# Windowed attention into a mixture of experts: v loaded once and shifted on chip, x's sums and rests on one engine

## The chip, the cores and the metric

One core of one Trainium2 chip runs the whole kernel in one launch. The metric is the device time in microseconds (us) of that launch. The engines are TensorE (PE), VectorE (DVE), ScalarE (ACT), GpSimd (POOL) and the queue of SyncE (SP), which issues every transfer.

## The reference, cut to what matters

q, k and v have the shape (4, 8, 576, 64); the mixture has 2304 tokens, model width 512, 8 experts and a hidden width of 1024. Everything is float32.

```python
scores = scale * np.matmul(q, k.transpose(0, 1, 3, 2))
rel = pos[:, None] - pos[None, :]
scores = np.where((rel >= 0) & (rel < 64), scores, -1e9)
attn = softmax(scores)                       # max subtracted, + 1e-9 in the sum
x = (attn @ v).transpose(0, 2, 1, 3).reshape(2304, 512)

logits = x @ w_gate;  P = np.exp(logits - logits.max())
for _ in range(8):                           # rows, then columns
    P /= P.sum(1, keepdims=True) + 1e-9
    P /= P.sum(0, keepdims=True) + 1e-9
    P *= N / E
for e in range(8):
    out += P[:, e:e+1] * (np.maximum(x @ w1[e], 0.0) @ w2[e])
```

## The kernel before, in words

**Attention.** The work goes in 16 pairs p of heads, four pairs to a batch entry. A pair has 9 blocks of 64 queries; a block sees its own 64 keys and the 64 before them. TensorE makes the scores of a pair, ACT copies the own half out of PSUM (`own`), VectorE merges in the half before and takes the row maximum (`merge`), POOL subtracts it (`shift`, L716), ACT takes the exponential (`exp`), VectorE the sum and its reciprocal (`soften`), POOL multiplies and writes each probability twice, side by side (`weigh`, L724). TensorE transposes the result (L321), VectorE masks the transposes into `p_t` (`turned`, L796), and TensorE multiplies by `v_win` (`mix`, L331). ACT copies the product into `x_raw` (`x_copy`, L553).

`v_win` holds for each block 128 rows of v: the own 64 keys on partitions 64 to 127 and the 64 before on partitions 0 to 63. So one pair's v is loaded twice, by L240 (288 KB) and, shifted by a block, by L241 (256 KB). It has two buffers; the load of pair p waits for the mix of pair p - 2.

**Order.** Each engine has its own list, written by hand, and works through it strictly in order. TensorE's turn p (`attend`) is the scores of p, the mix of p - 3 and the transposes of p - 2. POOL's turn p is `shift(p)`, `weigh(p - 1)`, and a piece of extra work. ACT's turn p is `exp(p - 1)`, `own(p)`, `x_copy(p - 3)`, and extra work. VectorE's is `turned(p - 3)`, `merge(p)`, `soften(p - 1)`, and extra work. SP issues q and k of pair p + 3, then v of pair p - 1, and in turns 4, 8 and 9 the weights of the first two tiles.

**The extra work.** The products x @ w1 are Strassen products in Winograd's form: seven (P1, P6, P2, P7, P5, P4, P3 in the order in which TensorE wants them) of quarter matrices. For x they need the sums T1 to T4 (`x_sum`, L705) beside P1, P2 and P3, which are parts of x itself. Each of the seven operands is split into a high part (`x_split`, a cast on ACT, L537) and a rest (`x_rest`, operand minus high part); likewise each tile of weights, with four sums (`sums`, L672 to L677), one split (`w1_split`, L520) and rests (`w1_rest`, L682). x comes in three superblocks s of 768 tokens: superblock 0 needs pairs 0 to 7 in full, and P1 and P2 of it only the first 384 tokens, which pairs 0 to 3 give. Here the rests of superblock 0 are made on VectorE (L817) in turns 12, 14, 15 and after, the sums T1 to T4 on POOL in turns 11 to 14, the sums of the first two weight tiles on POOL in turns 5 and 8.

**The seam.** After turn 16 TensorE does P1 and P6 of the first tile, turn 17 (mix of 14, transposes of 15), P2 and P7, the mix of 15, P5 and P4, the gate product over all of x, P3, and the transposes of the logits. From there 96 weight tiles (3 superblocks, 8 experts, 4 tiles each) run at TensorE's pace. On ACT the seam is: `exp(15)`, `x_copy(13)`, `p1_copy(0)`, the split of the second weight tile, `x_copy(14)`, `relu_11`, `x_copy(15)`, the other relus.

Of the kernel before, what the change touches and what calls it, by code (L numbers as in the profile page):

```python
# [12 lines left out]
P = 128  # L13
# [37 lines left out]
A11, A12, A22, S1, S2, S3, S4 = range(7)  # L51
OF_W = {P1: A11, P6: S2, P2: A12, P7: S3, P5: S1, P4: A22, P3: S4}
T1, T2, T3, T4 = range(4)
XRING = 10
BLK = 2 * P
RAW = 8 * BLK
# [2 lines left out]
def build(nc, qk, v, w_gate, w1, w2, consts, out):  # L59
    with ExitStack() as ctx:  # L60
# [78 lines left out]
        pads_set = sem("pads_set")  # L139
        qk_loaded = [sem(f"qk_loaded{i}") for i in range(QKR)]  # L140
        v_loaded = [sem(f"v_loaded{i}") for i in range(2)]
        scores_done = sem("scores_done")
        own_taken = sem("own_taken")
        scores_taken = sem("scores_taken")
# [84 lines left out]
        def _(sp):  # L229
# [6 lines left out]
            def load_v(p):  # L236

                if p >= 2:
                    sp.wait_ge(x_done, p - 1)
                sp.dma_start(v_win[WINDOW:P, p % 2, :, :], v[p]).then_inc(v_loaded[p % 2], 16)  # L240
                sp.dma_start(v_win[0:WINDOW, p % 2, 1:QB, :], v[p, :, 0:QB - 1, :]).then_inc(v_loaded[p % 2], 16)  # L241

            def load_w1(f, slot, done):

# [55 lines left out]
        def _(pe):  # L300
# [22 lines left out]
                last.then_inc(transposed, 1)  # L323

            def mix(p):
                pe.wait_ge(v_loaded[p % 2], (p // 2 + 1) * 32)
                pe.wait_ge(p_t_ready, p + 1)
                for i in range(QB):
                    for h in range(2):
                        c = slice(h * D, (h + 1) * D)  # L330
                        last = nc.tensor.matmul(ps_x[c, i * WINDOW:(i + 1) * WINDOW], v_win[:, p % 2, i, c],  # L331
                                                p_t[:, i, c], start=True, stop=True)
                last.then_inc(x_done, 1)
# [38 lines left out]
            def product(s, n, slot, k):  # L372

                x, y = bank[slot], bank[1 - slot]
                if k == P1:
                    pe.wait_ge(w1_lo_ready, n + 1)
                    wait(pe, h_ready, n * 4 - 1)
                    o, opens = x, True
                elif k == P6:
                    wait(pe, h_ready, n * 4)  # L380
                    o, opens = y, True
                elif k == P2:
                    pe.wait_ge(p1_out, n + 1)
                    o, opens = x, False
                elif k == P7:
                    pe.wait_ge(u2_done, n + 1)
                    o, opens = y, True
                elif k == P5:
                    pe.wait_ge(h_ready, n * 4 + 1)
                    o, opens = x, True  # L390
                elif k == P4:
                    pe.wait_ge(u3_done, n + 1)
                    o, opens = y, False
                else:
                    pe.wait_ge(h_ready, n * 4 + 2)
                    o, opens = x, True
                if s is not None:
                    pe.wait_ge(xv_lo_ready, s * PRODUCTS + k + 1)
                return o, opens

            def multiply(s, first, n, slot, k):
# [114 lines left out]
        def _(act):  # L516
# [11 lines left out]
            def x_split(s, k):  # L528
                if k in (P1, P2, P3):
                    if s == 0:  # L530
                        act.wait_ge(x_taken, 2 * PAIRS)
                else:
                    act.wait_ge(t_done, s * 4 + {P5: 1, P6: 2, P7: 3, P4: 4}[k])
                if s and k >= XRING - PRODUCTS:

                    act.wait_ge(prod_done, PRODUCTS * (s * PER_SB - 1) + (k - (XRING - PRODUCTS)) + 1)
                nc.scalar.copy(xv_hi[:, x_slot(s, k), :, :], x_operand(s, k)).then_inc(xv_hi_ready, 1)  # L537
# [6 lines left out]
            def own(p):  # L544
                act.wait_ge(scores_done, p + 1)
                wait(act, probs_ready, p - SCR + 1)
                nc.scalar.copy(sc[:, p % SCR, :, :], ps_s[:, :, WINDOW:KEYS]).then_inc(own_taken, 1)

            def x_copy(p):
                act.wait_ge(x_done, p + 1)  # L550
# [62 lines left out]
            for p in range(NP):  # L613
                if p:
                    exp(p - 1)
                own(p)
                if p >= 3:
                    x_copy(p - 3)
                if p == 6:
                    w1_split(0, 0, 0)  # L620
                if p == 11:
                    x_split(0, P1)
                if p == 13:
                    x_split(0, P6)
                    x_split(0, P2)
                if p == 14:
                    x_split(0, P7)
                    x_split(0, P5)
                if p == 15:
                    x_split(0, P4)  # L630
                    x_split(0, P3)
            exp(NP - 1)
            x_copy(NP - 3)
            p1_copy(0, 0)
            w1_split(1, 1, 0)
            x_copy(NP - 2)
# [25 lines left out]
        def _(pool):  # L662
# [30 lines left out]
            def x_sum(s, i):  # L693

                if s:
                    pool.wait_ge(xv_lo_ready, s * PRODUCTS)
                else:
                    pool.wait_ge(x_taken, 2 * PAIRS)
                b11, b12 = (x_raw[:, s, 0:2, h * HT:(h + 1) * HT] for h in range(2))
                b21, b22 = (x_raw[:, s, 2:4, h * HT:(h + 1) * HT] for h in range(2))  # L700
                if i in (T2, T4):
# [2 lines left out]
                        T4: (b21, t_raw[:, T2, :, :])}[i]  # L704
                nc.gpsimd.tensor_tensor(t_raw[:, i, :, :], a, b, ALU.subtract).then_inc(t_done, 1)  # L705

            def x_rest(s, k):
                pool.wait_ge(xv_hi_ready, s * PRODUCTS + k + 1)
                at = x_slot(s, k)
                nc.gpsimd.tensor_tensor(xv_lo[:, at, :, :], x_operand(s, k), xv_hi[:, at, :, :].bitcast(F32),  # L710
                                        ALU.subtract).then_inc(xv_lo_ready, 1)
# [19 lines left out]
            for p in range(NP):  # L731
                shift(p)
                if p:
                    weigh(p - 1)
                if p == 5:
                    sums(0, 0, 16)
                if 6 <= p < 11:
                    w1_rest(0, 0, p - 6, p - 5)
                if p == 8:
                    sums(1, 1, 16)  # L740
                if p == 10:
                    w1_rest(0, 0, 5, 7)
                if 11 <= p < 15:
                    x_sum(0, p - 11)
            weigh(NP - 1)
            w1_rest(1, 1)
            w2_rest(0, 0)
            sums(2, 0, landed(2))
# [43 lines left out]
        def _(dve):  # L792
# [14 lines left out]
            def soften(p):  # L807
# [2 lines left out]
                nc.vector.tensor_reduce(soft_sum[:, k, :], sc[:, k, :, :], AX_X, ALU.add).then_inc(sum_done, 1)  # L810
                dve.wait_ge(sum_done, p + 1)
                nc.vector.reciprocal(soft_inv[:, k, :], soft_sum[:, k, :]).then_inc(inv_done, 1)

            def x_rest(k):
                dve.wait_ge(xv_hi_ready, k + 1)
                at = x_slot(0, k)
                nc.vector.tensor_tensor(xv_lo[:, at, :, :], x_operand(0, k), xv_hi[:, at, :, :].bitcast(F32),  # L817
                                        ALU.subtract).then_inc(xv_lo_ready, 1)

            def rest(n, slot, o, f, half, i):  # L820
                dve.wait_ge(h_hi_ready, n * 4 + i + 1)
# [151 lines left out]
            for p in range(NP):  # L973
# [2 lines left out]
                merge(p)  # L976
                if p:
                    soften(p - 1)
                if p == 12:
                    x_rest(P1)  # L980
                if p == 14:
                    x_rest(P6)
                    x_rest(P2)
                if p == 15:
                    x_rest(P7)
                    x_rest(P5)
            turned(NP - 3)
            soften(NP - 1)
            x_rest(P4)
            x_rest(P3)  # L990
            add_u2(0, 0)
            turned(NP - 2)
            rest(0, 0, bank[0], 0, 0, 0)
# [76 lines left out]
```

## Time and profile before

| | us |
|---|---|
| median of 3 runs (lowest, highest) | 1644.83 (1643.73, 1647.8) |
| the profiled execution | 1645.22 |
| its span | 1643.3 |
| PE busy | 1600.0 |
| POOL busy | 995.5 |
| DVE busy | 744.2 |
| ACT busy | 526.7 |

Transfers of the attention stage, by line: q and k 576 KB a pair, median 9.5 us from issue to landing; v 288 KB a pair, 5.7 us, and 256 KB a pair, 8.1 us; weights 512 KB each.

Times of the trace count from the start of the span. The engines' busy times overlap, so they don't add up to the span. A row that ends in a bracket tells how long the engine sat idle before it, and what ended the idle time; "issue" there means that nothing in the profile shows what it waited for. The chain of waits follows the last instruction back to what released it. "PEclk" is the clock that the throttle granted to TensorE, as a part of full speed.

### The profile page before, as it was taken

Reading aid. Unit: us, or ns where it says so; the run is one execution under the profiler, and the core shown is the slowest. Engines: PE = TensorE matmul, PEld = TensorE weight load, DVE = VectorE, ACT = ScalarE, POOL = GpSimd, SP = SyncE. Lnnn points to the kernel's source line nnn. Section 1 sums busy time; section 2 is a strip of 40 time slices with the busy share of each in tenths; the row PEclk is TensorE's granted clock in tenths of the full one; section 3 lists DMA queues with packets and bytes.
Section 4 is the critical chain, followed back from the end, with each engine's and each line's share of the span. In section 5 each row is a group of like instructions: output and inputs, shape, how many; then the busy total and the mean of one; then the engine's idle time right before and its main releaser. Section 6 shows DMA issues by size and latency. Waiting matters only on the chain.

```text
span 1643.3 us, 24260 instructions
## 1 busy us (share of the span) xinstructions
PE 1600.0 (97%) x8880; PEld 1431.1 (87%) x8880; DVE 744.2 (45%) x1263; ACT 526.7 (32%) x753; POOL 995.5 (61%) x644
## 2 busy tenths in 40 slices
PE   7778999999999999999999999999999999999999
PEld 6667888888888888988888889888888898898888
DVE  5667734434344344344344344344344344344343
ACT  2432233233332333333323333334232333332321
POOL 4855455656656778566565565687655656656552
PEclk9989999999999999999999999999999999999999
DMA  8922112112122122121221211213212122121111
GB/s 232 223 67 77 51 53 78 60 68 77 51 77 71 56 77 98 70 77 51 77 75 53 77 56 72 77 51 102 88 54 77 54 74 77 51 77 71 57 64 38
DMA packets 35436, 124.58 MB, mean 76 GB/s; under 512 B 4160, under 2 KB 4416, under 8 KB 35392
## 3 DMA queue, kind: packets, MB, share of 16 engines
q1 hardware_dynamic: 35392, 123.99, 23.1%
q8 instruction: 28, 0.46, 0.1%
q14 instruction: 16, 0.13, 0.0%
HBM read 119.26 MB, written 4.72 MB: 75 GB/s over the span
## 4 chain that ended last, share of the span: by engine, by line
PE 93%; DVE 3%; POOL 2%; issue 1%; DMA 1%; ACT 0%; SPq 0%; POOLq 0%; DVEq 0%
PE ps L428 16%; PE ps L429 16%; PE ps L427 16%; PE ps L411 14%; PE ps L407 14%; PE ps L409 14%; PE ps L309 1%; DMA qk_buf<-qk 1%; POOL probs L724 1%; PE ps L321 1%; PE ps L331 1%; DVE xv_lo L817 0%; DVE row_sum L939 0%; POOL sc L716 0%; DVE p_t L796 0%
## 5 line engine op out<-in xcount | busy, mean ns | idle before, releaser
L682 POOL TENSOR_TENSOR w_lo<-w_raw,w_hi 128x1792 fp32r<-128x1792 f32 (+1 forms) x101 | 391.5, 3877 | 532.3 <-ACT w_hi L520 531.4
L562 ACT ACTIVATE h_hi<-ps 128x384 fp32r<-128x384 f32 x384 | 189.3, 493 | 961.5 <-DVE ps L841 450.4
L428 PE MATMUL ps<-w_lo,h_hi 128*128 128x512 f32 x1152 | 456.9, 397 | 0.0
L429 PE MATMUL ps<-w_hi,h_lo 128*128 128x512 f32 x1152 | 456.5, 396 | 0.0
L427 PE MATMUL ps<-w_hi,h_hi 128*128 128x512 f32 x1152 | 455.0, 395 | 1.3 <-POOL w_lo L689 1.3
L407 PE MATMUL ps<-xv_hi,w_hi 128*128 128x384 f32 x1344 | 450.8, 335 | 1.9 <-DVE h_lo L823 1.0
L411 PE MATMUL ps<-xv_hi,w_lo 128*128 128x384 f32 x1344 | 452.2, 336 | 0.0
L409 PE MATMUL ps<-xv_lo,w_hi 128*128 128x384 f32 x1344 | 449.9, 335 | 0.0
L823 DVE SCALAR_TENSOR_TENSOR h_lo<-ps,h_hi 128x384 fp32r<-128x384 f32 x384 | 214.2, 558 | 366.6 <-ACT h_hi L562 365.8
L407 PEld LDWEIGHTS ps<-xv_hi,w_hi 128*128 128x128 f32 x1344 | 253.4, 189 | 32.0 <-DVE h_lo L823 1.4
L409 PEld LDWEIGHTS ps<-xv_lo,w_hi 128*128 128x128 f32 x1344 | 253.2, 188 | 29.1
L429 PEld LDWEIGHTS ps<-w_hi,h_lo 128*128 128x128 f32 x1152 | 216.7, 188 | 50.3
L689 POOL TENSOR_TENSOR w_lo<-w_raw,w_hi 128x1024 fp32r<-128x1024 f32 x96 | 230.3, 2399 | 49.7 <-ACT w_hi L525 48.6
L411 PEld LDWEIGHTS ps<-xv_hi,w_lo 128*128 128x128 f32 x1344 | 253.0, 188 | 0.0
L427 PEld LDWEIGHTS ps<-w_hi,h_hi 128*128 128x128 f32 x1152 | 216.9, 188 | 24.6 <-POOL w_lo L689 1.6
L428 PEld LDWEIGHTS ps<-w_lo,h_hi 128*128 128x128 f32 x1152 | 216.9, 188 | 23.0
L520 ACT CAST w_hi<-w_raw 128x1792 fp32r<-128x1792 f32 x96 | 162.9, 1697 | 10.8 <-POOL w_raw L677 10.8
L829 DVE TENSOR_TENSOR u<-ps,p 128x384 f32<-128x384 f32 x96 | 53.5, 558 | 214.3 <-PE ps L411 205.1
L838 DVE TENSOR_TENSOR u<-ps,u 128x384 f32<-128x384 f32 x96 | 53.5, 558 | 139.2 <-PE ps L411 138.8
L525 ACT CAST w_hi<-w_raw 128x1024 fp32r<-128x1024 f32 x96 | 99.9, 1041 | 0.0
L834 DVE TENSOR_TENSOR u<-ps,u 128x384 f32<-128x384 f32 x96 | 53.5, 557 | 102.2 <-PE ps L411 102.2
L861 DVE SCALAR_TENSOR_TENSOR x_raw<-ps,prob,x_raw 128x512 f32<-128x512 f32 x126 | 92.1, 744 | 9.8 <-PE ps L429 9.8
(74 smaller groups left out, 949.9 us busy)
## 6 DMA issues: line engine op xcount, KB each, us to landing
w_raw<-w SPq DMA_DIRECT2D x192, 512.0 KB, 3.9
qk_buf<-qk SPq DMA_DIRECT2D x16, 576.0 KB, 9.5
v_win<-v SPq DMA_DIRECT2D x16, 288.0 KB, 5.7
out<-x_raw SPq DMA_DIRECT2D x18, 256.0 KB, 2.3
v_win<-v SPq DMA_DIRECT2D x16, 256.0 KB, 8.1
const_sb<-consts SPq DMA_DIRECT2D x1, 176.0 KB, 3.5
wg<-w_gate SPq DMA_DIRECT2D x1, 64.0 KB, 5.5
```

The costliest lines, as they stand in the source:

```text
L407: nc.tensor.matmul(o, w1_hi[:, slot, c], xv_hi[:, at, kk, :], start=(opens and kk == 0), stop=False, skip_group_check=not opens)
L409: nc.tensor.matmul(o, w1_hi[:, slot, c], xv_lo[:, at, kk, :], start=False, stop=False, skip_group_check=not opens)
L411: last = nc.tensor.matmul(o, w1_lo[:, slot, c], xv_hi[:, at, kk, :], start=False, stop=(kk == 1), skip_group_check=not opens)
L427: nc.tensor.matmul(ps_y[t], h_hi[slot][:, f, c], w2_hi[slot][:, f, :], start=opens, stop=False)
L428: nc.tensor.matmul(ps_y[t], h_hi[slot][:, f, c], w2_lo[slot][:, f, :], start=False, stop=False)
L429: last = nc.tensor.matmul(ps_y[t], h_lo[slot][:, f, c], w2_hi[slot][:, f, :], start=False, stop=closes)
L520: nc.scalar.copy(w1_hi[:, slot, :], w1_raw[:, slot, BLK:RAW]).then_inc(w1_hi_ready, 1)
L525: nc.scalar.copy(w2_hi[slot][:].rearrange("p f d -> p (f d)"), w2_raw[:, slot, :])\
L562: nc.scalar.activation(h_hi[slot][:, f, half * HT:(half + 1) * HT], o, ACT.Relu)\
L682: last = nc.gpsimd.tensor_tensor(w1_lo[:, slot, c], w1_raw[:, slot, (lo + 1) * BLK:(hi + 1) * BLK], w1_hi[:, slot, c].bitcast(F32), ALU.su ...
L689: nc.gpsimd.tensor_tensor(w2_lo[slot][:].rearrange("p f d -> p (f d)"), w2_raw[:, slot, :], w2_hi[slot][:].rearrange("p f d -> p (f d)").b ...
L823: nc.vector.scalar_tensor_tensor(h_lo[slot][:, f, c], o, 0.0, h_hi[slot][:, f, c].bitcast(F32), ALU.max, ALU.subtract).then_inc(h_ready, 1)
```

## The change

- SP no longer issues L241. ACT gets `v_shift(p)`: it copies blocks 0 to 7 of `v_win` from partitions 64 to 127 to blocks 1 to 8 on partitions 0 to 63, once v of pair p has landed and the mix of p - 2 is done. It stands behind `x_copy(p - 1)` in turn p + 2; the mix of p waits for it.
- The rests of superblock 0 leave VectorE and go to POOL. P1 and P2 are split in turns 7 and 8, from the first four pairs, and their rests made in turns 8 and 9. T1 to T4 are in turns 10, 11, 13 and 15, the rests of P5 and P6 in turns 12 and 14, those of P7, P3 and P4 after the last `weigh`.
- The sums of the first weight tile go from turn 5 to 3, its rest from turns 6 to 10 to turns 4 to 6 in two, two and three blocks. The sums of the second tile go from turn 8 to behind the last rest of x.
- The probabilities are written twice, as before.

```diff
@@ the order in which the rests of superblock 0 come ready
+X_TURN = [P1, P2, P5, P6, P7, P3, P4]
@@ SP
                 sp.dma_start(v_win[WINDOW:P, p % 2, :, :], v[p]).then_inc(v_loaded[p % 2], 16)
-                sp.dma_start(v_win[0:WINDOW, p % 2, 1:QB, :], v[p, :, 0:QB - 1, :]).then_inc(v_loaded[p % 2], 16)
@@ TensorE, mix and product
-                pe.wait_ge(v_loaded[p % 2], (p // 2 + 1) * 32)
+                pe.wait_ge(v_loaded[p % 2], (p // 2 + 1) * 16)
+                pe.wait_ge(v_shifted, p + 1)
...
-                    pe.wait_ge(xv_lo_ready, s * PRODUCTS + k + 1)
+                    pe.wait_ge(xv_lo_ready, s * PRODUCTS + (k if s else X_TURN.index(k)) + 1)
@@ ACT
-                        act.wait_ge(x_taken, 2 * PAIRS)
+                        act.wait_ge(x_taken, 2 * PAIRS if k == P3 else PAIRS)
...
+            def v_shift(p):
+                act.wait_ge(v_loaded[p % 2], (p // 2 + 1) * 16)
+                wait(act, x_done, p - 1)
+                nc.scalar.copy(v_win[0:WINDOW, p % 2, 1:QB, :], v_win[WINDOW:P, p % 2, 0:QB - 1, :])\
+                  .then_inc(v_shifted, 1)
...
                 if p >= 3:
                     x_copy(p - 3)
-                if p == 6:
+                if p >= 2:
+                    v_shift(p - 2)
+                if p == 4:
                     w1_split(0, 0, 0)
-                if p == 11:
-                    x_split(0, P1)
-                if p == 13:
-                    x_split(0, P6)
-                    x_split(0, P2)
-                if p == 14:
-                    x_split(0, P7)
-                    x_split(0, P5)
-                if p == 15:
-                    x_split(0, P4)
-                    x_split(0, P3)
+                if p in (7, 8):
+                    x_split(0, (P1, P2)[p - 7])
+                if 11 <= p < 15:
+                    x_split(0, (P5, P6, P3, P7)[p - 11])
             exp(NP - 1)
+            x_split(0, P4)
+            v_shift(NP - 2)
             x_copy(NP - 3)
+            v_shift(NP - 1)
             p1_copy(0, 0)
             w1_split(1, 1, 0)
             x_copy(NP - 2)
@@ POOL
-            def x_rest(s, k):
-                pool.wait_ge(xv_hi_ready, s * PRODUCTS + k + 1)
+            def x_rest(s, k, nth=0):
+                pool.wait_ge(xv_hi_ready, s * PRODUCTS + (nth or k + 1))
...
-                    pool.wait_ge(x_taken, 2 * PAIRS)
+                    pool.wait_ge(x_taken, PAIRS + 2 if i == T1 else 2 * PAIRS)
...
-                if p == 5:
+                if p == 3:
                     sums(0, 0, 16)
-                if 6 <= p < 11:
-                    w1_rest(0, 0, p - 6, p - 5)
+                if 4 <= p < 7:
+                    w1_rest(0, 0, (0, 2, 4)[p - 4], (2, 4, 7)[p - 4])
                 if p == 8:
-                    sums(1, 1, 16)
+                    x_rest(0, P1, 1)
+                if p == 9:
+                    x_rest(0, P2, 2)
                 if p == 10:
-                    w1_rest(0, 0, 5, 7)
-                if 11 <= p < 15:
-                    x_sum(0, p - 11)
+                    x_sum(0, T1)
+                if p == 11:
+                    x_sum(0, T2)
+                if p == 12:
+                    x_rest(0, P5, 3)
+                if p == 13:
+                    x_sum(0, T3)
+                if p == 14:
+                    x_rest(0, P6, 4)
+                if p == 15:
+                    x_sum(0, T4)
             weigh(NP - 1)
+            x_rest(0, P7, 6)
+            x_rest(0, P3, 6)
+            x_rest(0, P4, 7)
+            sums(1, 1, 16)
             w1_rest(1, 1)
             w2_rest(0, 0)
@@ VectorE: x_rest and its calls in turns 12, 14, 15 and after the last soften are gone
```

## Rows read from the trace of the kernel before

**Rows 1.** The page, busy us, share of the span and instructions of each engine

```profile
PE 1600.0 (97%) x8880; PEld 1431.1 (87%) x8880; DVE 744.2 (45%) x1263; ACT 526.7 (32%) x753; POOL 995.5 (61%) x644
```

**Rows 2.** Stretches: length; PE, PEld, DVE, ACT, POOL busy; PEclk, DMA share, GB/s

```profile
60.00:70.00 10.00, 7.70 (x138) 6.95 (x135) 7.37 (x10) 4.04 (x8) 9.82 (x9) 1.00 1.04 232
...
90.00:100.00 10.00, 4.30 (x45) 3.82 (x45) 9.93 (x9) 2.69 (x4) 6.96 (x4) 0.66 0.22 56
```

**Rows 3.** The chain of waits in the attention stage: start, us, what

```profile
70.32 2.94 issue
...
86.74 4.61 DVE xv_lo L817 x2
...
96.09 2.86 DVE xv_lo L817
```

**Rows 4.** TensorE in order of time: start, us, operation, idle before

```profile
15.99 3.56 PE L309 MATMUL ps<-qk_buf 64*64 64x64 f32 x36 [4.07 <-DMA qk_buf<-qk]
...
21.70 2.08 PE L309 MATMUL ps<-qk_buf 64*64 64x64 f32 x36 [1.02 <-DMA qk_buf<-qk]
...
26.46 2.08 PE L309 MATMUL ps<-qk_buf 64*64 64x64 f32 x36
...
30.80 2.08 PE L309 MATMUL ps<-qk_buf 64*64 64x64 f32 x36
...
114.44 1.27 PE L331 MATMUL ps<-p_t,v_win 128*64 128x64 f32 x36 [1.48 <-DVE p_t L796]
```

**Rows 5.** A stretch of half a microsecond, columns as in rows 2

```profile
103.50:104.00 0.50, 0.50 (x5) 0.50 (x4) 0.50 (x1) 0.00 (x0) 0.42 (x1) 0.50 0.84 203
```

**Rows 6.** POOL in order of time

```profile
26.18 1.15 POOL L716 TENSOR_TENSOR sc<-sc,row_max 128x576 f32<-128x576 f32 x1 [1.02 <-DVE row_max L805]
...
38.46 0.73 POOL L672 TENSOR_TENSOR w_raw<-w_raw 128x256 f32<-128x256 f32 x1
...
41.33 1.15 POOL L716 TENSOR_TENSOR sc<-sc,row_max 128x576 f32<-128x576 f32 x1
...
81.64 1.15 POOL L716 TENSOR_TENSOR sc<-sc,row_max 128x576 f32<-128x576 f32 x1 [3.23 <-PE ps L321]
82.75 2.11 POOL L724 TENSOR_TENSOR probs<-sc,soft_inv 128x1152 f32<-128x1152 f32 x1
84.83 1.82 POOL L705 TENSOR_TENSOR t_raw<-x_raw 128x768 f32<-128x768 f32 x1
86.60 1.15 POOL L716 TENSOR_TENSOR sc<-sc,row_max 128x576 f32<-128x576 f32 x1
...
101.21 2.70 POOL L724 TENSOR_TENSOR probs<-sc,soft_inv 128x1152 f32<-128x1152 f32 x1 [3.08 <-DVE soft_inv L812]
```

**Rows 7.** The page's groups: busy, mean ns of one, idle before

```profile
L689 POOL TENSOR_TENSOR w_lo<-w_raw,w_hi 128x1024 fp32r<-128x1024 f32 x96 | 230.3, 2399 | 49.7 <-ACT w_hi L525 48.6
...
L525 ACT CAST w_hi<-w_raw 128x1024 fp32r<-128x1024 f32 x96 | 99.9, 1041 | 0.0
```

**Rows 8.** ACT in order of time

```profile
81.08 0.84 ACT L537 CAST xv_hi<-t_raw 128x768 fp32r<-128x768 f32 x1
...
105.82 1.69 ACT L520 CAST w_hi<-w_raw 128x1792 fp32r<-128x1792 f32 x1
109.77 0.65 ACT L553 COPY x_raw<-ps 128x576 f32<-128x576 f32 x1 [2.26 <-PE ps L331]
111.95 0.49 ACT L562 ACTIVATE h_hi<-ps 128x384 fp32r<-128x384 f32 x1 [1.54 <-PE ps L411]
```

**Rows 9.** Transfers issued from 67 to 69 us, then from 85 to 88

```profile
v_win<-v SPq DMA_DIRECT2D x1, 288.0 KB, 7.5
...
v_win<-v SPq DMA_DIRECT2D x1, 288.0 KB, 3.5
```

**Rows 10.** VectorE in order of time

```profile
101.05 0.90 DVE L817 TENSOR_TENSOR xv_lo<-t_raw,xv_hi 128x768 fp32r<-128x768 f32 x1
```

**Rows 11.** SP's queue in order of time

```profile
102.60 1.43 SPq L241 DMA_DIRECT2D v_win<-v  x1
```

More of the change, by code:

```diff
@@ L141, in build @@
         v_loaded = [sem(f"v_loaded{i}") for i in range(2)]
+        v_shifted = sem("v_shifted")
         scores_done = sem("scores_done")
@@ L812, in soften @@
                 nc.vector.reciprocal(soft_inv[:, k, :], soft_sum[:, k, :]).then_inc(inv_done, 1)
[L814 to L818, printed above, removed]
             def rest(n, slot, o, f, half, i):
@@ L978, in _ @@
                     soften(p - 1)
[L979 to L986, printed above, removed]
             turned(NP - 3)
             soften(NP - 1)
-            x_rest(P4)
-            x_rest(P3)
             add_u2(0, 0)
```

## The prediction, made before the changed kernel ran

> **What bounds the kernel now.** The page first: TensorE is busy 97% of the span [rows 1], so the long part of the kernel, the 96 weight tiles of the mixture, can't be shortened by this change, which touches none of it. All edits lie before the first gate product, in the first 118 us, and only a shift of that point counts. Next I read the stretches of that part [rows 2]: in 60 to 70 us the DMA engines are busy all the time, and in 90 to 100 us they are not, VectorE is (9.93 of 10 us), and TensorE is at 4.30 of 10 with a mean granted clock of 0.66. Third, the chain of waits [rows 3]: it has a wait of 2.94 us at 70.32 ahead of a probabilities-times-v product, with no releaser named (a copy of v that hasn't landed), and then VectorE's rests of x, 4.61 us and 2.86 us, ahead of the masking of the transposed probabilities. So two things hold the attention stage back: v's transfers up to about 80 us, VectorE's rests from 86 us. Without either, a pair takes 4.34 us (26.46 to 30.80), TensorE's own work back to back; from 30.80 to the last pair's mix at 114.44 the trace is far from that [rows 4].
>
> **The change, part by part.**
>
> *The second copy of v goes.* It is 256 KB (262,144 bytes) in each of 16 pairs. While a copy of v is what moves, the engines are 0.84 busy at 203 GB/s [rows 5], which is 242 GB/s at full share, so one costs 1.1 us of DMA time, or 1.3 at 203. Two of them are ahead of qk of pair 2 or 3 at the start: the third score block waits for its data until 15.99 and the fourth starts at 21.70 [rows 4]. With one copy less in front, 1.3 us at 203 GB/s, the third starts near 14.6; the fourth has two less, and what it waits for then is the scores buffer and not data: 5.1 us after the third, near 19.7 (3.6 of the third's own work, 0.6 and 0.8 of copy and merge, and gaps), 2.0 us earlier. I shift all that follows by 2.0: the subtraction of the row maximum of pair 3 on POOL from 26.18 [rows 6] to 24.15. From there DMA has slack: 864 KB a pair are 3.8 us at 232 GB/s against periods of 4.3 and more.
>
> *The shift on ACT.* Sixteen copies of 64x1024 elements. No such copy is in the trace; the nearest row on ACT is the cast of 128x1024 at 1.04 us [rows 7], which I take. Bounds: 0.65 us, the 576-element copy of the same engine [rows 8], and 2.40 us, POOL's two-input operation of 128x1024 [rows 7]. It stands in order behind the copy of x, and behind it waits the next exponential, hence the normalising and POOL's weighing. ACT does 0.6 + 0.6 + 0.6 of copies and exponential in a pair and now 1.0 more (and 0.8 in six pairs for a split of x): under 3.9 us of 4.3 to 5 (the split of x: [rows 8]). It also waits for v. The kept copy of v landed 3.5 us after issue at 85 us and 7.5 at 67 us [rows 9]. It is issued at the end of a mix and the shift comes a period and a copy of x later, at 5.0 to 5.6 us, so a landing of about 4 costs nothing; with w_2's 512 KB in front, 1 to 2 us more, the 1.2 us that ACT has to spare take it. Cost taken: 0.
>
> *x's sums and rests on POOL.* This sets the pace. POOL's steady loop from the rows of one pair [rows 6]: subtraction 81.64 to 82.75, weighing to 84.83, one x operation of 128x768 to 86.60: 1.11 + 2.08 + 1.77 = 4.96 us. The rests have the same shape and two inputs, so 1.77 each. After the change every pair from 8 to 15 has one. Starts of the subtraction on POOL, worked forward from 24.15: pair 3 also takes the four weight sums (2.87, from 38.46 to 41.33), 6.1 us, so pair 4 at 30.3; its exponential waits for the 1.7 us split of the weights on ACT, pair 5 at 34.85 and pair 6, with two blocks of rest, at 39.3; three blocks (1.77) put pair 7 at 44.3; pair 8 comes after TensorE's 4.35 at 48.65; then seven periods of 4.96 with x_rest P1 first: pair 15 at 83.4. Its weighing of pair 14, the last sum T4, and the last weighing, from 88.4 to 90.4. Before, the last one began at 101.21 [rows 6]: 12.8 us sooner.
>
> *What VectorE loses.* Seven rests, which lay on the chain for 7.5 us of the 12.8 above. One took 0.90 where it began just ahead of POOL's weighing at 101.21 [rows 10, 6], and another 2.86 on the chain [rows 3].
>
> The Trainium skill, GPSIMD Engine Reference, section 3.1, says that a two-input operation costs GpSimd about twice what it costs VectorE, and keeps elementwise work on VectorE. By 0.90 against 1.77 the rows agree on the ratio; they don't show VectorE as the cheaper place, since there it took up to 2.86. By the page alone the move would add 7 x 0.9 = 6 us to the pacing engine; the sum above has it in the 4.96.
>
> *The tail.* After the last weighing POOL now does three rests (5.3 us) and the four sums of the second weight tile (2.87), which before were done at pair 8. They end at 90.4 + 8.2 = 98.6. ACT's split of that tile waits for them, and behind it in ACT's order stand the copy of x of pair 14, the first relu and what follows. From the rows [rows 8]: split 1.6, copy 0.6, so relu at 100.9; before, from the relu at 111.95 to the last mix at 114.44 it was 2.49. The last mix is at 103.3 instead of 114.44: 11.1 us sooner. The other arm (P1 and P6 after the transposes of pair 14 at 87.9, x_split P4 after T4 at 89.1, both v shifts, copy for P1, mix of 14, P2) would have allowed the relu by about 98.8, so the late sums eat 2.1 to 2.5 us of the gain. Behind the mix all is as before: P5, P4, gate, logits; POOL's weight rest ends near 104, well ahead of the next tile.
>
> **Sum.** The profiled execution took 1645.22 us (span 1643.3 and 1.9 around it), 0.4 above the median of 1644.83. 1645.2 - 11.1 = 1634.1; against the median, 1633.7. I say 1634.
>
> **The rivals.**
>
> *A, the tail doesn't hold.* If the mix isn't held by the sums, the gain is 13.3 and the time 1631. For: the split is early on ACT's list. Against: the order is fixed in both lists. 7%.
>
> *B, v's transfers still bind.* If the removed half runs beside the kept one rather than after it, the kept one lands as late as now and the stage keeps its waits to pair 13 at 81.64; then two POOL periods, the last weighing at 96.5 instead of 88.4, 8.1 us of the gain gone: 1642. For: the halves go to different partitions. Against: in [rows 5] one copy was in flight (the other's issue lasted from 102.60 to 104.03 [rows 11]) and the engines were 0.84 busy, not half. The Trainium skill, DMA: Bandwidth & Descriptors, section The descriptor swizzle, has partitions 64 to 127 served by engines 8 to 15 and the others by 0 to 7 in a 128-partition transfer; carried over to these copies it would give this rival, and 0.84 speaks against it. 6%.
>
> *C, slower: v arrives late for ACT.* The shift is in ACT's order; with landing L after issue, the shift and the exponential behind it give a period of (L + 3.1)/2 (issue 1.27 after the scores' end, shift 1.04, exponential and scores copy next). It passes 4.96 at L = 6.8, and all of the 11.1 us are gone over 13 pairs when the period is 5.8, at L = 8.5. The steady landings of before reach 7.5 [rows 9], with both copies in the queue. At L = 9.5 in every pair it is 6.3: 1634 + 17 = 1651. A shift of 2.40 us (the upper bound) alone gives 5.95 in the six pairs with a split: 1640. 6% for this, 5 of them slower.
>
> *D, POOL is slowed.* Beside VectorE's two-input rests a weighing took 2.70 instead of 2.11 (101.21 against 82.75, [rows 6]). I count none after, since those rests are gone. If the eight of pairs 8 to 15 take 2.70 for other reasons, 8 x 0.59 = 4.7: 1639; if the rests and sums are slowed as well, 1641. 5%.
>
> **How the numbers follow.** Forecast 76%, A 7, B 6, C 6, D 5. A measurement of this kernel can tell 0.3%, 4.9 us, from no change: faster means under 1639.9. The forecast and A are faster, 3 of D too; B, the rest of D and 1 of C are within; 5 of C slower: 0.86, 0.09, 0.05. Range: POOL's sum is a floor, so little lies under A: 1630.5. Small waits of 0.1 to 0.3 a period on 12 pairs add up to 3.6; TensorE after an idle stretch showed a clock of 0.5 (the third score block took 3.56 us, others 2.08 [rows 4]), and if it is low again for the last mix, P5, P4 and the gate, 3 us more: 1640.5.
>
> **What would show it.** Right: one DMA of v a pair, landing near 4 us; v shifts of about 1.04 us; POOL over 95% busy from pair 8 on with starts 4.96 apart; the last weighing near 88 us, ACT idle before the second weight split on POOL's sums, the gate at 107. Wrong: waits of ACT or TensorE for v (C, B), weighings of 2.7 (D), the last mix before 101.5 (A), or periods over 5.3 with POOL idle in them, which none of my cases has.

## The result and the profile after

The changed kernel took 1632.88 us (median of 6 runs, 1631.9 to 1633.29) against 1643.93 (6 runs, 1639.35 to 1647.8): ratio 0.994, 95% interval 0.9928 to 0.9951. Run again beside the last experiments it was 1634.12 against 1642.70: 0.9952 (0.9934 to 0.9969). So the gain is 8.6 to 11.1 us; the forecast was 1634, 11.1 under the profiled 1645.2.

The changed kernel's page, busy time by engine, and then two groups of its transfers over the first 100 us (count, size, median us to landing):

```profile
PE 1594.6 (98%) x8880; PEld 1426.4 (87%) x8880; DVE 730.7 (45%) x1256; ACT 543.0 (33%) x769; POOL 1003.8 (62%) x648
```

```profile
qk_buf<-qk SPq DMA_DIRECT2D x16, 576.0 KB, 5.6
v_win<-v SPq DMA_DIRECT2D x16, 288.0 KB, 5.1
```

The stretches that answer to [rows 2], same columns, of the changed kernel:

```profile
60.00:70.00 10.00, 7.70 (x126) 6.80 (x126) 6.91 (x10) 6.96 (x12) 9.18 (x7) 1.00 0.69 184
80.00:90.00 10.00, 6.46 (x90) 5.65 (x85) 4.62 (x7) 4.74 (x7) 10.00 (x7) 1.00 0.38 105
90.00:100.00 10.00, 6.06 (x57) 5.66 (x57) 1.82 (x2) 3.52 (x5) 8.11 (x8) 0.83 0.02 8
```

The DMA engines are no longer full at 60 us (0.69 for 1.04). In 80 to 90 us POOL has no gap at all, and in 90 to 100 VectorE does 1.82 us for 9.93.

POOL in order of time, which answers to [rows 6]: a start of the row-maximum subtraction (L724), two whole periods, the one gap, and the end.

```profile
23.20 1.16 POOL L724 TENSOR_TENSOR sc<-sc,row_max 128x576 f32<-128x576 f32 x1 [1.63 <-PE ps L323]
...
52.28 1.16 POOL L724 TENSOR_TENSOR sc<-sc,row_max 128x576 f32<-128x576 f32 x1
53.38 2.12 POOL L732 TENSOR_TENSOR probs<-sc,soft_inv 128x1152 f32<-128x1152 f32 x1
55.46 1.83 POOL L718 TENSOR_TENSOR xv_lo<-x_raw,xv_hi 128x768 fp32r<-128x768 f32 x1
57.23 1.16 POOL L724 TENSOR_TENSOR sc<-sc,row_max 128x576 f32<-128x576 f32 x1
...
62.18 1.16 POOL L724 TENSOR_TENSOR sc<-sc,row_max 128x576 f32<-128x576 f32 x1
...
68.02 1.15 POOL L724 TENSOR_TENSOR sc<-sc,row_max 128x576 f32<-128x576 f32 x1 [0.82 <-DVE row_max L827]
...
82.89 1.18 POOL L724 TENSOR_TENSOR sc<-sc,row_max 128x576 f32<-128x576 f32 x1
...
87.85 2.14 POOL L732 TENSOR_TENSOR probs<-sc,soft_inv 128x1152 f32<-128x1152 f32 x1
```

Pairs 9, 10 and 11, at 52.28, 57.23 and 62.18, are 4.95 apart: the period of 4.96 that was added up. Of pairs 9 to 15 only pair 12, at 68.02, comes later than that, 5.84 after pair 11. The last weighing starts at 87.85 for 101.21 before. ACT shows why pair 12 is late, and what its shift of v costs:

```profile
16.67 1.04 ACT L556 COPY v_win<-v_win 64x1024 f32<-64x1024 f32 x1
...
57.36 1.04 ACT L556 COPY v_win<-v_win 64x1024 f32<-64x1024 f32 x1 [1.05 <-DMA v_win<-v]
...
63.29 1.04 ACT L556 COPY v_win<-v_win 64x1024 f32<-64x1024 f32 x1 [2.57 <-DMA v_win<-v]
```

These two waits, for v of pairs 8 and 9, are the only ones of over 0.3 us for v in the stage. The copies of pairs 8, 9 and 10 landed 6.4, 7.7 and 7.2 us after issue, with w2's loads in the queue; those after them took 3.6 to 3.8. Behind the second wait ACT has the exponential of pair 11 and the scores copy of pair 12, and so pair 12 is late on POOL.

The chain of waits at the seam, from the last weighing's end:

```profile
90.00 5.30 POOL xv_lo L718 x3
95.30 0.68 POOL w_raw L680
...
98.19 1.70 ACT w_hi L523
99.89 0.53 ACT x_raw L563
100.41 0.40 ACT h_hi L572
...
101.31 1.36 DVE p_t L818
102.67 0.14 issue
102.80 1.27 PE ps L334 x36
```

That is the tail as it was worked out: three rests, four sums (the first is shown, the last starts at 97.42), the split of the second weight tile, and the last mix at 102.80.

### The profile page after: what moved, and what is told of

Read it like the earlier page. It is cut to its first block, busy times and chain, and to the rows that moved or that the text cites. A ratio compares the mean times of both kernels' runs of the same rounds, so it can differ in the third digit from the quotient of the medians.

```text
span 1631.0 us, 24286 instructions
## 1 busy us (share of the span) xinstructions
PE 1594.6 (98%) x8880; PEld 1426.4 (87%) x8880; DVE 730.7 (45%) x1256; ACT 543.0 (33%) x769; POOL 1003.8 (62%) x648
## 4 chain that ended last, share of the span: by engine, by line
PE 92%; POOL 4%; DVE 2%; issue 1%; ACT 0%; DVEq 0%; POOLq 0%
PE ps L431 16%; PE ps L432 16%; PE ps L430 16%; PE ps L414 14%; PE ps L410 14%; PE ps L412 14%; POOL probs L732 2%; POOL sc L724 1%; POOL xv_lo L718 1%; DVE prob L980 0%; POOL t_raw L713 0%; DVE row_sum L955 0%; PE ps L311 0%; PE ps L477 0%; PE ps L323 0%
## 5 line engine op out<-in xcount | busy, mean ns | idle before, releaser
L690 POOL TENSOR_TENSOR w_lo<-w_raw,w_hi 128x1792 fp32r<-128x1792 f32 (+2 forms) x98 | 391.0, 3990 | 528.8 <-ACT w_hi L523 528.0
```

Source lines behind the costliest of these rows:

```text
L690: last = nc.gpsimd.tensor_tensor(w1_lo[:, slot, c], w1_raw[:, slot, (lo + 1) * BLK:(hi + 1) * BLK], w1_hi[:, slot, c].bitcast(F32), ALU.su ...
```

## The experiments

Each was timed beside the kernel before on the same chip, in three groups. The medians of before were 1642.13 (e1_v_once, e2_two_loads, e3_sums_sooner, e4_w2_late), 1642.19 on another chip (e6_shift_twice to e9_seam_more) and 1642.70 (e10_seam_w2, before_again, after_again). Each median is compared with the one beside it. The changed kernel itself was timed beside before at ratios 0.994 and 0.9952; where an experiment is compared with it, the ratios are compared. In a diff "..." stands for lines that are not shown.

### One half of the change at a time

```diff
--- before
+++ e1_v_once: the second load goes, v_shift comes, all else as before
-                sp.dma_start(v_win[0:WINDOW, p % 2, 1:QB, :], v[p, :, 0:QB - 1, :]).then_inc(v_loaded[p % 2], 16)
...
+                if p >= 2:
+                    v_shift(p - 2)
...
+            v_shift(NP - 2)
             x_copy(NP - 3)
+            v_shift(NP - 1)
```

> The kernel before with only v's part of the change: one load of v, the shift on ACT; sums and rests where they were. My theory (v's transfers held the stage up to 80 us, VectorE's rests after it): the row-maximum subtraction of pair 13 on POOL starts near 74.2 instead of 81.64, and the rests on VectorE then cost what they did; 7.4 us less, 1636.5 us (1635 to 1639). Rival (the transfers were covered, and all of the gain comes from the rests): within 2 us of the kernel before.

Measured: 1640.51 us (1639.1 to 1642.33), ratio 0.999 (0.9981 to 0.9999), 1.6 us sooner. My 7.4 was far too much, and by the median alone the rival (within 2 us of before) came true. In its trace the stage did speed up; POOL in order of time, then ACT:

```profile
75.52 1.15 POOL L728 TENSOR_TENSOR sc<-sc,row_max 128x576 f32<-128x576 f32 x1
...
88.08 1.15 POOL L728 TENSOR_TENSOR sc<-sc,row_max 128x576 f32<-128x576 f32 x1 [1.18 <-DVE row_max L817]
...
95.09 2.70 POOL L736 TENSOR_TENSOR probs<-sc,soft_inv 128x1152 f32<-128x1152 f32 x1 [3.07 <-DVE soft_inv L824]
```

```profile
99.88 1.05 ACT L554 COPY v_win<-v_win 64x1024 f32<-64x1024 f32 x1 [2.77 <-DMA v_win<-v]
100.84 0.47 ACT L567 COPY p<-ps 128x384 f32<-128x384 f32 x1
```

Pair 13 is at 75.52 (74.2 expected; 81.64 before), the last weighing at 95.09, 6.1 us sooner. Then the last v, issued when the mix of 13 ends at 96.48, is what ACT waits for until 99.88, and the copy of P1, on which TensorE waits, is behind it. At the rest of the first w_2 tile on POOL 5.1 us are left (120.77 for 125.83). The profiled execution took 1639.6 us, near its median; the two traced executions of the kernel before (below) took 1645.2 and 1644.7, above theirs. So the traces overstate the difference, by up to 3 and 1 us. Why the medians differ by 1.6 and not by 5.1 I can't show.

```diff
--- after
+++ e2_two_loads: v loaded twice again, no v_shift; x's work as in the changed kernel
...
+                sp.dma_start(v_win[0:WINDOW, p % 2, 1:QB, :], v[p, :, 0:QB - 1, :]).then_inc(v_loaded[p % 2], 16)
...
-                if p >= 2:
-                    v_shift(p - 2)
...
```

> The changed kernel with v loaded twice again and no shift on ACT: only x's sums and rests moved. My theory: waits for v as before up to pair 13 at about 81 us, then two POOL periods, last weighing near 96: 1641 us (1639 to 1643), so a gain of some 3 of the 11 us. Rival (the second load costs nothing once x's work is on POOL): 1633, as the changed kernel.

Measured: 1641.43 us (1634.57 to 1645.5), ratio 0.9997 (0.9985 to 1.0009). The time is the theory's, but it had counted from 1645: beside before the gain is 0.7 us and not 3, and can't be told from none. POOL:

```profile
73.46 1.15 POOL L720 TENSOR_TENSOR sc<-sc,row_max 128x576 f32<-128x576 f32 x1 [3.29 <-DVE row_max L823]
...
79.79 1.15 POOL L720 TENSOR_TENSOR sc<-sc,row_max 128x576 f32<-128x576 f32 x1 [1.33 <-DVE row_max L823]
...
94.67 2.12 POOL L728 TENSOR_TENSOR probs<-sc,soft_inv 128x1152 f32<-128x1152 f32 x1
```

With both copies in the queue POOL stands idle 3.29 us before pair 12 and 1.33 before pair 13, and the last weighing is at 94.67 for 87.85: the stage is as the theory had it (about 81 for pair 13, 96 for the last weighing).

How do the halves add up? In the traces, against the kernel before, in us sooner:

| | e1_v_once | e2_two_loads | both (the changed kernel) |
|---|---|---|---|
| last weighing on POOL | 6.1 | 6.5 | 13.4 |
| last mix | 5.1 | 4.8 | 11.6 |
| rest of w2's first tile | 5.1 | 3.4 | 10.1 |
| medians | 1.6 | 0.7 | 8.6 to 11.1 |

In the attention stage the halves add, within the scatter (the second trace of the changed kernel, below, has 12.2 for 13.4): two delays that follow each other on one chain, each taken away by one half. At the seam each half alone loses some: e1_v_once waits for the last v as above, and e2_two_loads has the late sums (split of the second weight tile at 105.03, last mix at 109.65), by which the whole change loses 1.8 us too. The medians show much less for each half alone than the traces do; with one trace of each, that difference stays open.

### VectorE or POOL for the rests

```diff
--- after
+++ e7_rests_dve: x_rest back on VectorE, POOL's calls gone
...
+                if p in (8, 9, 12, 14):
+                    x_rest({8: P1, 9: P2, 12: P5, 14: P6}[p], {8: 1, 9: 2, 12: 3, 14: 4}[p])
             turned(NP - 3)
             soften(NP - 1)
+            x_rest(P7, 6)
+            x_rest(P3, 6)
+            x_rest(P4, 7)
```

> The changed kernel with the seven rests of x of superblock 0 back on VectorE, in the same turns as they have on POOL in the changed kernel (8, 9, 12, 14 and after the last reciprocal). Theory: POOL's turns without an x operation fall from 4.96 to TensorE's 4.35 (4 x 0.6 less), collisions of the rests with POOL's work give most of it back (a rest of up to 2.9 us holds VectorE, a weighing takes 2.7 instead of 2.1), and after the last weighing the sums come 5.3 us sooner but TensorE's P2 holds the relu: 1631.5 (1630 to 1634). Rival (the gain of the change comes from having the rests off VectorE at all): 1637 or more. Rival (VectorE is the better place, 0.9 us each): 1629 or less.

Measured: 1631.76 us (1630.83 to 1634.16), ratio 0.9937 (0.992 to 0.9953): as the changed kernel, within what can be told. VectorE and then POOL in its trace:

```profile
80.21 1.22 DVE L828 TENSOR_TENSOR xv_lo<-t_raw,xv_hi 128x768 fp32r<-128x768 f32 x1
...
87.51 0.90 DVE L828 TENSOR_TENSOR xv_lo<-t_raw,xv_hi 128x768 fp32r<-128x768 f32 x1
88.33 2.58 DVE L828 TENSOR_TENSOR xv_lo<-x_raw,xv_hi 128x768 fp32r<-128x768 f32 x1
90.99 2.70 DVE L828 TENSOR_TENSOR xv_lo<-t_raw,xv_hi 128x768 fp32r<-128x768 f32 x1
```

```profile
80.57 2.83 POOL L732 TENSOR_TENSOR probs<-sc,soft_inv 128x1152 f32<-128x1152 f32 x1
84.28 1.15 POOL L724 TENSOR_TENSOR sc<-sc,row_max 128x576 f32<-128x576 f32 x1 [0.88 <-DVE row_max L816]
```

A rest on VectorE takes 0.90 to 2.70 us (1.7 in the mean of seven), and the weighing beside it 2.83 for 2.12. A pair with a rest takes 4.82 us (79.46 to 84.28) for 4.96, but the one behind it up to 5.4, so that from pair 8 to pair 15 it is 35.1 us for the changed kernel's 35.6, of which 0.9 are its late pair 12. So the move to POOL is not what brought the gain. Before, six of the seven rests stood in turn 14 and later, three of them on the chain of waits for 7.5 us; here four stand in turns 8 to 14. What is left as the cause is this order of the lists. No run separates it from the other moves that both kernels share, those of the weight sums and of T1 to T4.

### How much room ACT has

```diff
--- after
+++ e6_shift_twice: each shift done twice, and the mix waits for both
...
                 nc.scalar.copy(v_win[0:WINDOW, ...], v_win[WINDOW:P, ...]).then_inc(v_shifted, 1)
+                act.wait_ge(v_shifted, 2 * p + 1)
+                nc.scalar.copy(v_win[0:WINDOW, ...], v_win[WINDOW:P, ...]).then_inc(v_shifted, 1)
```

> The changed kernel with v's shift done twice in a row on ACT for each pair (the second copy waits for the first, same data): 1.04 us more of ACT a pair. Theory (ACT has 1.0 to 1.2 us to spare in a pair, less the 0.8 us of a split of x in six of them): the six pairs with a split go from 4.96 to about 5.6 us, the others stay; 3 to 5 us more, 1637 (1635 to 1639). Rival (ACT's shift is wholly covered, even twice): 1633. Rival (ACT is the bound already): 16 x 1.04 more, 1649.

Measured: 1635.06 us (1632.6 to 1636.16), ratio 0.9955 (0.9939 to 0.9972). The time is in the range, the place isn't. POOL's periods stay 4.96 (68.14, 73.11, 78.07, 83.04) and the last weighing is at 88.00:

```profile
78.07 1.15 POOL L727 TENSOR_TENSOR sc<-sc,row_max 128x576 f32<-128x576 f32 x1
...
83.04 1.14 POOL L727 TENSOR_TENSOR sc<-sc,row_max 128x576 f32<-128x576 f32 x1
```

ACT is nearly full there (4.9 us in a pair with a split), but its copies of x only come later, and POOL's starts don't move. One pair is longer, pair 7 (5.00 for 4.11), where POOL has no x operation, and the gap ahead of pair 12 is not there in this trace. At the seam the second shifts do show: the copy of P1 starts at 93.51 for 91.24, the first relu at 101.51 for 100.31. But by the gate product nothing is left of it (107.52, for 107.86 and 107.48 in the two traces of the changed kernel), and the ratio can't be told from the changed kernel's. So the shift, costed at nothing, has 1 us of cover in nearly all pairs, and doubling it costs nothing that these runs can tell.

### The seam

```diff
--- after
+++ e3_sums_sooner
             x_rest(0, P7, 6)
+            sums(1, 1, 16)
             x_rest(0, P3, 6)
             x_rest(0, P4, 7)
-            sums(1, 1, 16)
```

> The changed kernel with the four sums of the second weight tile ahead of the rests of P3 and P4 on POOL, so they end 3.5 us sooner. My theory: the seam is held by these sums, but only until TensorE's P2 (done near 98.7 in the changed kernel's trace) holds the first relu instead of 100.3: 1.6 us less, 1631.3 (1630 to 1632.3). Rival 1: the whole 3.1 us come, 1629.8. Rival 2: the seam isn't held by the sums, no change, 1632.9.

Measured: 1632.54 us (1629.95 to 1633.21), ratio 0.9939 (0.9927 to 0.9952), against 0.994 and 0.9952 of the changed kernel: no difference that can be told. Its trace has the effect that the theory named:

```profile
95.17 1.69 ACT L523 CAST w_hi<-w_raw 128x1792 fp32r<-128x1792 f32 x1 [2.93 <-POOL w_raw L685]
96.76 0.63 ACT L563 COPY x_raw<-ps 128x576 f32<-128x576 f32 x1
99.37 0.49 ACT L572 ACTIVATE h_hi<-ps 128x384 fp32r<-128x384 f32 x1 [1.97 <-PE ps L414]
```

The split is 3.0 us sooner (95.17 for 98.19), and the relu then waits for TensorE's P2, 0.9 us sooner than in the changed kernel.

```diff
--- after
+++ e8_seam
@@ ACT
             exp(NP - 1)
-            x_split(0, P4)
-            v_shift(NP - 2)
             x_copy(NP - 3)
-            v_shift(NP - 1)
+            v_shift(NP - 2)
             p1_copy(0, 0)
-            w1_split(1, 1, 0)
+            x_split(0, P4)
+            v_shift(NP - 1)
             x_copy(NP - 2)
             relu_11(0, 0)
             x_copy(NP - 1)
+            w1_split(1, 1, 0)
@@ VectorE
-            add_u2(0, 0)
             turned(NP - 2)
+            add_u2(0, 0)
```

> The changed kernel with two orders changed at the seam. ACT: after the last exponential the copy of x of pair 13, v's shift of 14, the copy of P1, the split of P4, v's shift of 15, the copy of x of 14, the relu, the copy of x of 15, and only then the split of the second weight tile. VectorE: the masking of pair 14 before the sum u2. Theory (the late sums and P1's copy behind T4 and v's shifts hold the seam, nothing behind it needs that split for 10 us): mix of 14 at 89.5 instead of 93.8, mix of 15 near 95 instead of 102.8: 7 to 8 us less, 1625 (1623 to 1628). Rival (something else in the seam comes right behind, P4's rest or the weight rest on POOL): 2 us less, 1631.

Measured: 1625.65 us (1624.29 to 1627.93), ratio to before 0.9901 (0.9883 to 0.9919): 16.5 us under before, and by the ratios (0.9901 for 0.994 and 0.9952) 6.4 to 8.4 under the changed kernel. The chain of waits:

```profile
89.22 1.20 PE ps L334 x36
90.42 1.13 PE ps L323 x9
...
92.65 0.50 ACT h_hi L572
...
93.65 1.36 DVE p_t L818
95.14 1.27 PE ps L334 x36
```

The mix of 14 is at 89.22 and the last mix at 95.14, as expected (89.5, 95). The last weighing is where it was, at 87.62. So two waits were 7.7 us of the seam, and the order of two engines' lists was all of it: 4.6 us up to the mix of 14 (P1's copy on ACT behind T4's split and both shifts, and the masking behind the sum u2 on VectorE), 3.0 us behind it (the split behind the late sums). The edits were made together; the parts are read from this one trace.

```diff
--- e8_seam
+++ e9_seam_more: the loads of w2 as in e10_seam_w2 below, and on POOL
-                if p == 15:
-                    x_sum(0, T4)
             weigh(NP - 1)
             x_rest(0, P7, 6)
+            x_sum(0, T4)
```

> As e8_seam, and also: T4 on POOL behind the last weighing and the rest of P7, so the last weighing comes 1.8 us sooner; both loads of w2 behind the last load of v, so v is in time for pairs 9 and 10 (0.8 us). Theory: the mix of 14 was ready at 89.5 in e8_seam's expectation and the transposes of 15 right behind it, so the sooner weighing gives about 1 us, the loads 0.8: 1623 (1621 to 1626). Rival (T4's later place makes P4's rest late and holds P4 and the gate): no better than e8_seam.

Measured: 1628.01 us (1625.39 to 1628.44), ratio 0.9908 (0.989 to 0.9927): no better than e8_seam, which was the rival's number. To tell T4's place from that of the loads, the loads were moved alone, with T4 where it was in e8_seam:

```diff
--- e8_seam
+++ e10_seam_w2
-                if p == 8:
-                    load_w2(0, 0, 0)
-                if p == 9:
-                    load_w2(1, 1, 0)
             load_v(NP - 1)
+            load_w2(0, 0, 0)
+            load_w2(1, 1, 0)
```

> e8_seam and only the loads of w2 moved behind the last load of v (T4 stays where it was). Theory: the idle 0.8 us on POOL before pair 12 goes, and nothing else changes: 1625.0 (1624 to 1626.5). Rival (the later loads cost as much elsewhere, as e9_seam_more came out 2.4 us over e8_seam): 1627 to 1628. If it is 1625 here, what made e9_seam_more slower is T4's place.

Measured: 1626.65 us (1624.68 to 1627.89), ratio 0.9902 (0.9882 to 0.9922), the same as e8_seam. The same edit on the changed kernel alone (its expectation has the landings one pair off: the waits of 1.05 and 2.57 belong to landings of 6.4 and 7.7, of pairs 8 and 9, and not 9 and 10 as e9_seam_more's has it):

> The changed kernel with both loads of w2 issued after the last load of v instead of in turns 8 and 9. In the changed kernel's trace v landed 7.7 and 7.2 us after issue there, ACT waited 1.05 and 2.57 us for it, and POOL stood idle 0.8 us before pair 12. Theory: that 0.8 us comes back, 1632.1 (1631.5 to 1632.6), v lands within 5.5 us in every pair. Rival: the idle time has another cause, no change.

Measured: 1633.59 us (1631.65 to 1635.94), ratio 0.995 (0.9938 to 0.9962): the 0.8 us are not to be seen in a median. In its trace POOL's gap is gone (pair 11 at 64.08, pair 12 at 69.03). But e8_seam, with the loads in turns 8 and 9, has no gap there either (62.81, 67.76), though ACT waits 0.78 and 1.49 us for v; so e10_seam_w2 had nothing to win back. The three traces with the gap (after, after_again, e3_sums_sooner) have a wait for v of 2.57, 2.46 and 2.70. Late v makes the gap, then, when it is late enough, and w2's loads don't make it so late in every execution.

T4's place can be read from the traces. From the mix of 14 to the last mix it is 5.99 us in e8_seam, e10_seam_w2 and e9_seam_more alike, and 3.5 from there to the gate: T4's later place held nothing back, so the rival had the number and not the cause. It could bring nothing either: in e8_seam the transposes of 15 start at 90.35, right behind the mix of 14, when the last weighing is already over (87.62 and 2.12). The mix of 14 itself is later in both kernels with moved loads (91.98 and 91.26 for 89.15), behind transposes and first products at half clock (products 0.32 us apart, not 0.18), which stand behind the same idle times as in e8_seam (1.8 and 0.7 us). Why the clock fell there isn't shown.

### What varies by itself

> The kernel before, unchanged, for a second trace. Its profiled execution took 1645.2 us, but the medians beside the experiments were 1642.1 and 1642.2. Theory (the stage bound by v's transfers varies from execution to execution, and so does the third score block, at half clock in one trace): median within 1 us of 1642.2, and a last weighing on POOL up to 3 us off 101.21. Rival (the stage is the same in every execution and the scatter comes after 130 us): last weighing within 0.5 us of 101.21.

> The changed kernel, unchanged, on the same chip as before_again, for a ratio of medians from one place and a second trace. Theory: 1632.9 (1631.5 to 1634), 9 to 11 us under before_again; last weighing on POOL within 1 us of 87.85.

Measured: before_again 1643.81 us (1641.06 to 1647.08), ratio 1.0006 (0.9994 to 1.0018); after_again 1634.12 (1631.99 to 1638.2). The last weighing of before_again on POOL, and the rest of w2's first tile:

```profile
100.45 2.70 POOL L724 TENSOR_TENSOR probs<-sc,soft_inv 128x1152 f32<-128x1152 f32 x1 [3.07 <-DVE soft_inv L812]
...
125.84 2.36 POOL L689 TENSOR_TENSOR w_lo<-w_raw,w_hi 128x1024 fp32r<-128x1024 f32 x1 [14.25 <-ACT w_hi L525]
```

and of after_again:

```profile
89.02 2.14 POOL L732 TENSOR_TENSOR probs<-sc,soft_inv 128x1152 f32<-128x1152 f32 x1
...
115.38 2.36 POOL L697 TENSOR_TENSOR w_lo<-w_raw,w_hi 128x1024 fp32r<-128x1024 f32 x1 [10.27 <-ACT w_hi L528]
```

At that last point the two traces of before agree to 0.01 us and the two of the changed kernel to 0.4 (115.74, 115.38), though their last weighings differ by 0.8 and 1.2. That they agree to 0.01 is in part chance: in before_again the mix of pair 13 came 0.75 us sooner but ran at half clock to its end (2.19 us for 1.70), and by the mix of 14 the two are level (108.47, 108.46). The gain there is 10.1 and 10.5 us. What follows to the end of the span varies more: 1517.5 and 1516.0 us before, 1515.3 and 1516.9 after. All of that arises before 200 us: from the fifth w2 rest (198.64 in before) to the last of the 96, the distance between any two of these traces changes by less than 0.1 us.

So the last weighing fits neither my theory's 3 us nor the rival's 0.5; that the scatter lies behind 130 us, the rival's other half, is so in these traces. Both medians came out over their ranges (1643.81 for 1642.2 and 1 us, 1634.12 for at most 1634), and after_again's last weighing was 1.17 us off for at most 1; its 9.7 us under before_again are as expected.

## Why the prediction was right

**What holds the stage.** Right in the traces: v's transfers, then VectorE's rests, two delays in a row. Taken away singly they brought the last weighing forward by 6.1 and 6.5 us, together by 13.4 (12.2 in after_again), for the 12.8 forecast. The medians of the halves (1.6 and 0.7 us) are smaller than that, and why is open.

**v's transfers.** The third score block started at 13.86 for a forecast of 14.6, the fourth at 18.72 for 19.7, pair 3 on POOL at 23.20 for 24.15. The third block took 2.08 us, not the 3.56 of before, which I had kept. The lead was 1.0 us at pair 3 and 1.3 at pair 8. With the 0.9 of pair 12 against it, the last weighing came out 0.5 from the forecast: two misses that nearly cancel, which is luck.

**The shift on ACT.** 1.04 us each, hidden in the pairs (e6_shift_twice). The claim that ACT's spare 1.2 us would take the 1 to 2 us of w2's loads failed in one pair: with landings of 6.4 and 7.7 us ACT waited 1.05 and 2.57, and POOL lost 0.8. That is rival C's mechanism, on both sides of its 6.8, and no more of it. C's other price, 5.95 us a pair from a shift of 2.40, isn't added up from any row; with 2.08 us of shift e6_shift_twice kept 4.96 to 5.00 in all pairs with a split.

**POOL's pace.** 4.96 added up, 4.95 measured. Last weighing 88.4 against 87.85.

**What VectorE loses.** The saving is real, the reason too narrow: the rests on VectorE cost as much where they stood, in turns 14, 15 and after. In e7_rests_dve, spread as in the changed kernel, they cost no more on VectorE than on POOL. One rest there took the 0.90 of the rows; the others took 1.22 to 2.70, and a weighing beside them 2.83, so little was left of VectorE's advantage. The rule of the Trainium skill's GPSIMD Engine Reference, section 3.1, that a two-input operation is about twice as dear on GpSimd, would have made that kernel the faster one. The trace agrees where VectorE's operation isn't held up (0.90 for 1.77); for the kernel the measurement decides, and it shows no difference that can be told (0.9937 for 0.994 and 0.9952).

**The tail.** The last mix at 103.3 was forecast, 102.80 measured, behind the sums as said. Behind it I had all as before; it wasn't. P5 and P4 ran at half clock, as the range had allowed, and cost 1.6 us. In after_again they did not: the gate is 3.5 us behind the last mix there (103.98, 107.48), so this is one execution's clock and not the change's. TensorE in order of time:

```profile
102.80 1.27 PE L334 MATMUL ps<-p_t,v_win 128*64 128x64 f32 x36 [2.96 <-DVE p_t L818]
...
104.44 0.53 PE L412 MATMUL ps<-xv_lo,w_hi 128*128 128x384 f32 x1
...
107.86 0.63 PE L343 MATMUL ps<-x_raw,wg 128*32 128x512 f32 x3
```

The gate is 5.1 us behind the last mix for 3.5 before. So 10.1 us of the 11.6 were left there. The span is 12.3 us shorter, 2.2 more. By w2's rests on POOL 0.7 of them came between 138 and 154 us and 1.5 between 176 and 199 (times of before), in the Sinkhorn steps (the normalisation by rows and columns), where TensorE waits for VectorE (busy 1.7 of 5 us) and its granted clock then falls. The same stretch, shifted by 10.1 us, of before and then of the changed kernel:

```profile
180.00:185.00 5.00, 5.00 (x15) 4.42 (x16) 2.41 (x9) 0.00 (x0) 0.88 (x2) 0.50 0.42 164
```

```profile
169.90:174.90 5.00, 5.00 (x20) 4.15 (x20) 3.08 (x9) 0.12 (x1) 0.24 (x1) 0.76 0.23 94
```

A mean granted clock of 0.50 for 0.76 over 5 us. In the second pair it is the other way round, 0.68 in before_again and 0.50 in after_again, and what follows the last common point is 0.9 us longer in the changed kernel, so this is scatter and not the change. That the median came out 1.1 us from 1634 owes something to such scatter: the two pairs of medians give 11.1 and 8.6 us.

**The rivals.** A (the tail doesn't hold) is refuted by the chain; the 2 us it promised are not what the seam had to give, which e8_seam puts at 6 to 8, since I took the copy of P1 behind T4 and both shifts as given. (Its own sum is off by one: 1645.2 less 13.3 is 1632, not 1631.) B is refuted: pair 13 started at 72.97 and not at 81.64, v landed at 3.6 to 3.8 us from pair 11 on, and DMA share fell to 0.69. D is refuted: weighings took 2.12.

## What to carry to other kernels

Where two causes of delay lie one after the other on one chain, look at a common point of the traces for what each removal brings (6.1 and 6.5 us alone, 13.4 together here), and then at the seam behind it for what each loses again; the medians alone (1.6, 0.7, and 8.6 to 11.1) would have hidden the first. Add up the turn of the engine that will be the pace next, row by row, and then follow each engine's list through the seam to the next stage: instructions that nobody needs yet, standing ahead of one on the chain and waiting for another engine's late work, cost 6 to 8 us here. And move work off an engine only after asking whether it could stand elsewhere in that engine's own list.

## What the runs showed of the hardware

A copy on ACT from partitions 64 to 127 to partitions 0 to 63 of 1024 elements took 1.04 us, the same as a cast of 128x1024 that stays on its partitions. A 288 KB copy landed 3.6 us after issue, and 7.7 with two loads of 512 KB issued in the two turns before. A two-input operation of 128x768 took 0.90 to 2.70 us on VectorE with POOL at work, and a POOL operation of 128x1152 beside it 2.83 us for 2.12. And the third score block took 2.08 us behind gaps of 2.0 to 2.3 us in nine traces, 2.62 behind 2.75 (granted clock 0.77 over it), 3.64 and 3.56 behind 2.98 and 4.07 (0.57 over the last), but 2.08 behind 3.22 in e2_two_loads: in these traces the block was dearer behind the longer idle stretches, but not every time.
